# Attention and two feed-forward layers on one core: identity products in TensorE's prologue taken out

## What is computed

```python
q_d, k_d, v_d = means of q, k, v over groups of 4 positions
out_up    = repeat(softmax(scale * q_d @ k_d.T) @ v_d, 4)
scores    = where(|i - j| < 4, scale * q @ k.T, -1e9)
out_local = softmax(scores) @ v
x = (out_up + out_local) as (2304 tokens, 512)
h = relu(x @ w_in1)                 # 512 -> 2048
x = (h * h) @ w_out1                # 2048 -> 512
h = x @ w_in2
out = (relu(h) + log1p(exp(-|h|))) @ w_out2
```

## Time and profile before

| | |
|---|---|
| three runs | 908.38 to 908.83 us, median 908.71 |
| the profiled execution | 910.32 us, its span 908.5 us |
| TensorE matmul busy | 890.9 us, 98% of the span |
| VectorE, ScalarE, GpSimd busy | 612.3, 440.1 and 331.0 us |
| granted TensorE clock, mean | 0.988 of full |
| HBM read and written | 54.76 and 9.44 MB |

### The profile page before, as it was taken

One profiled execution on the slowest core, in us unless ns is written; L12 is line 12 of the kernel. 1 busy time (PEld: TensorE's weight loads), 2 busy tenths in 40 slices (PEclk: granted clock), 3 DMA queues, 4 the chain that ended last, 5 costly groups with the idle time before them and its releaser, 6 DMA issues.

```text
span 908.5 us, 14912 instructions
## 1 busy us (share of the span) xinstructions
PE 890.9 (98%) x5783; PEld 834.5 (92%) x5783; DVE 612.3 (67%) x1058; ACT 440.1 (48%) x1073; POOL 331.0 (36%) x160
## 2 busy tenths in 40 slices
PE   9979899999999999999999999999999999999998
PEld 7778799999999999999999999998999989999897
DVE  4579776876676766645245977777767767677675
ACT  5576355554646446453466634434434434434433
POOL 8699868788585975856100000000000000000000
PEclk9689999999999999999999999999999999999999
DMA  9670231231424221100155400200200200200000
GB/s 302 254 286 28 70 137 59 65 113 70 138 84 137 68 83 46 45 27 1 45 158 166 127 0 1 70 1 1 70 1 1 71 1 0 70 1 1 36 1 35
DMA packets 22037, 65.14 MB, mean 72 GB/s; under 512 B 2272, under 2 KB 9440, under 8 KB 21968
## 3 DMA queue, kind: packets, MB, share of 16 engines
q1 hardware_dynamic: 21968, 64.20, 21.0%
HBM read 54.76 MB, written 9.44 MB: 71 GB/s over the span
## 4 chain that ended last, share of the span: by engine, by line
PE 87%; POOL 6%; issue 2%; DVE 2%; ACT 1%; DMA 1%; SPq 0%; POOLq 0%; DVEq 0%
PE bank L1267 22%; PE bank L1281 22%; PE bank L680 20%; PE bank L649 20%; POOL w_lo L709 3%; POOL prod L451 2%; POOL prod L405 1%; PE bank L545 1%; DMA qk_first<-in_qk_grp 1%; PE bank L590 1%; PE bank L472 1%; PE bank L615 1%; PE bank L288 1%; DVE xs L482 0%; ACT bank L565 0%
## 5 line engine op out<-in xcount | busy, mean ns | idle before, releaser
L649 PE MATMUL bank<-x_hi,w_hi 128*128 128x288 f32 x512 | 157.6, 308 | 4.9 <-DVE g_lo L669 3.1
L451 POOL TENSOR_TENSOR prod<-sc,vt 128x1344 f32<-128x1344 f32 x42 | 134.9, 3235 | 60.0 <-DVE sc L439 52.4
L669 DVE TENSOR_TENSOR g_lo<-bank,g_hi 128x288 fp32r<-128x288 f32 x128 | 58.3, 456 | 144.5 <-ACT g_hi L664 144.4
L649 PE MATMUL bank<-x_lo,w_hi 128*128 128x288 f32 x512 | 152.2, 297 | 0.0
L649 PE MATMUL bank<-x_hi,w_lo 128*128 128x288 f32 x512 | 152.0, 297 | 0.0
L680 PE MATMUL bank<-g_hi,w_hi 128*128 128x288 f32 x512 | 150.9, 295 | 0.0
L680 PE MATMUL bank<-g_hi,w_lo 128*128 128x288 f32 x512 | 150.7, 294 | 0.0
L680 PE MATMUL bank<-g_lo,w_hi 128*128 128x288 f32 x512 | 150.6, 294 | 0.0
L995 ACT ACTIVATE sp_abs<-bank 128x384 f32<-128x384 f32 x96 | 46.9, 489 | 194.4 <-PE bank L1267 194.3
L405 POOL TENSOR_TENSOR prod<-qt,kt 128x1344 f32<-128x1344 f32 x42 | 130.7, 3118 | 17.9 <-DVE sc L412 12.3
L1267 PE MATMUL bank<-x_lo,w_hi 128*128 128x384 f32 x384 | 129.9, 338 | 0.0
(11 more groups left out here) (104 smaller groups left out, 1623.5 us busy)
## 6 DMA issues: line engine op xcount, KB each, us to landing
w_raw<-in_w SPq DMA_DIRECT2D x32, 512.0 KB, 4.2
qk<-in_qk_grp SPq DMA_DIRECT2D x12, 576.0 KB, 4.6
kt<-in_k_loc SPq DMA_DIRECT2D x7, 960.0 KB, 4.9
vt<-in_v_loc SPq DMA_DIRECT2D x7, 960.0 KB, 4.7
vg<-in_v_grp SPq DMA_DIRECT2D x16, 320.0 KB, 3.5
x_scratch<-ys SPq DMA_DIRECT2D x32, 144.0 KB, 3.1
x_raw<-x_scratch SPq DMA_DIRECT2D x6, 768.0 KB, 4.6
out<-y SPq DMA_DIRECT2D x18, 256.0 KB, 2.0
```

The lines of the kernel that those rows point to most:

```text
L451: nc.gpsimd.tensor_tensor(dst, pb, win, ALU.mult).then_inc(prod_ready[m % 2], 1)
L649: last = nc.tensor.matmul(h_ps[f % 2][:, 0:NT], w[:, f, wc], x[:, T % 2, kc], start=(kc == 0 and i == 0), stop=(kc == KC - 1 and i == 2))
L669: nc.vector.tensor_tensor(g_lo[:, f % 2], h_ps[f % 2][:, 0:NT], g_hi[:, f % 2].bitcast(F32), ALU.subtract).then_inc(g_ready, 1)
```

## The change

`keep_busy` and all its calls are taken out, and with them the argument `busy` of `first_x`. Every other instruction keeps its place in its engine's list. Since `first_x` had its fillers behind the waits for `x0_ready` and `up_ready`, those waits now stand directly before its own. In the changed file, code behind the function stands 5 or 6 lines higher.

```diff
@@ -282,11 +282,6 @@
             a.wait_ge(mask0_done, 2)
             nc.scalar.activation(mask0_r[0:BQ], mask0[0:BQ], ACT.Copy).then_inc(mask0_rounded, 1)
 
-        def keep_busy(pe, times):
-
-            for _ in range(times):
-                nc.tensor.matmul(X0[:, 0:P], ident[:], ident[:], start=True, stop=True)
-
         def first_scores(pe, j):
             pe.wait_ge(first_qk[j], 16)
             if j >= 2:
@@ -353,13 +348,12 @@
             for e in range(2):
                 nc.vector.tensor_copy(pT0[0:BK, j % 2, e], first_banks(j)[e][0:BK, 0:NT]).then_inc(pT0_copied, 1)
 
-        def first_x(pe, j, busy):
+        def first_x(pe, j):
 
 
             if j:
                 pe.wait_ge(x0_ready, j)
                 pe.wait_ge(up_ready, j)
-            keep_busy(pe, busy)
             if j == 0:
                 pe.wait_ge(v0_loaded, 16)
             pe.wait_ge(pT0_copied, 2 * j + 2)
@@ -1197,36 +1191,28 @@
         def _(pe):
             pe.wait_ge(ident_done, 2)
 
-            keep_busy(pe, 7)
             first_scores(pe, 0)
-            keep_busy(pe, 3)
             pair_scores(pe, 0)
-            keep_busy(pe, 6)
             first_scores(pe, 1)
-            keep_busy(pe, 4)
             first_turn(pe, 0)
-            keep_busy(pe, 1)
             pair_scores(pe, 1, (0,))
-            keep_busy(pe, 4)
             first_scores(pe, 2)
-            keep_busy(pe, 2)
             pair_turn(pe, 0)
-            keep_busy(pe, 3)
             pair_scores(pe, 1, (1,))
-            first_x(pe, 0, 5)
+            first_x(pe, 0)
             first_turn(pe, 1)
             pair_turn(pe, 1)
             pair_scores(pe, 2)
             first_scores(pe, 3)
             first_turn(pe, 2)
             pair_scores(pe, 3, (0,))
-            first_x(pe, 1, 0)
+            first_x(pe, 1)
             pair_turn(pe, 2)
             pair_scores(pe, 3, (1,))
             first_turn(pe, 3)
-            first_x(pe, 2, 4)
+            first_x(pe, 2)
             pair_turn(pe, 3)
-            first_x(pe, 3, 5)
+            first_x(pe, 3)
 
             hidden_in(pe, 0, 0)
             hidden_in(pe, 0, 1)
```

## The result

The changed kernel took 913.06 us in the median of 6 runs (912.01 to 914.64), the kernel before 908.41 us in 6 runs beside it (905.83 to 908.83). The ratio is 1.0053, interval 1.0034 to 1.0071: slower by 4.6 us, where 3.3 were forecast. The profiled execution took 912.71 us, its span is 910.9 us, 2.4 us longer than the span of before.

The account below looks back on a forecast made before the run. TensorE is packed from about 105 us, so prologue delay arrives whole. Steps after 10.2 us sum to 37.85 us, so `first_x(3)` ends at 48.0 instead of 44.7: 908.7 + 3.3 = 912.0 us, range 909.2 to 914.6.

Parts of the forecast that it names:

- The clock stays low without the early fillers: Prologue: with nothing dense before the hidden layer, TensorE's clock is low from 0; `first_turn(3)` comes 7 us late.
- Rival B: About even: clock rises once on scores of pair 2 and `first_scores(3)`; end at -1.5 to +0.8, 908.5 us; chance 0.12.
- The chain of steps: TensorE's prologue steps and copy waits after 10.2 us, at low clock: 37.85 us, `first_x(3)` ends at 48.0 instead of 44.7.
- The low start of the hidden layer (3 us) is paid before and after alike: Start of the hidden layer: 3 us at low clock in both kernels, so no difference from it.
- truly full about 3 us into the hidden layer: Sign in the changed kernel: TensorE's clock first reaches full about 3 us after the hidden layer begins.
- rival C: Slower: hidden layer stays low longer than 3 us, until 62 instead of about 51 us; +3 more, 915 us; chance 0.11.
- Late fillers "stand on the path" and only cost: Fillers in the low stretch: 2.0 us before `first_x(2)`, 2.4 us before `first_x(3)`, partly covering waits.
- Early fillers cost little at full clock: Prologue fillers at full clock fill time in which TensorE would wait for DMA, VectorE or ScalarE anyway.
- One for one downstream: After `first_x(3)`: its 3.3 us delay passes through VectorE's chain to 71.14 us and arrives at TensorE's end.
- the forecast 74.4: Sign in the changed kernel: GpSimd's first value product comes at 74.4 us, 71.14 before.
- The size: Whole kernel: +3.3 us, profiled execution from 910.32 to 913.6, median from 908.7 to 912.0 us.
- The rule on keeping TensorE busy: Skill rule: unbroken work reaches full clock; by it the prologue's real work raises it, -4 to -6, 904 us; chance 0.06.

Follow-up runs that it names:

- e3_first_seven: Only the first 7 of the 44 fillers left, at the head of TensorE's list, against the kernel before: 912.81 us, ratio 1.0036.
- e1_late_out: The 9 fillers at the heads of `first_x(2)` and `first_x(3)` out, 35 earlier ones kept, against the kernel before: 908.58 us, ratio 0.9993.
- e8_half: e5_hold with 24 early fillers in place of 35, measured against the kernel before: 904.21 us, ratio 0.9970.
- e5_again: e5_hold's kernel run once more to confirm it, against the kernel before: 905.03 us, ratio 0.9967.
- the second comparison: The changed kernel, all 44 fillers out, run once more beside the kernel before: 914.44 us, ratio 1.0049.
- e6_sixteen: Only the first 16 fillers (7, 3 and 6, up to `first_scores(1)`) left, against the kernel before: 912.01 us, ratio 1.0033.
- e5_hold: The 9 late fillers out, 35 early ones kept, 7 others put where TensorE stood idle, against the kernel before: 906.44 us, ratio 0.9967.

## Why the prediction was right, step by step

- **The clock stays low without the early fillers: right** in the trace and in 17 of 18 timed runs of the changed kernel, by their times (912 us or more). Rival B, given 0.12, is what the eighteenth did, and e3_first_seven's trace shows it too.
- **The chain of steps: right, 48.0 us forecast, 47.56 measured.** The single heads of the pair scores at low clock measure 1.07 to 1.17 us from start to start, where 1.13 was taken between 0.63 and 1.34. `first_scores` is 1.89, not 1.83: the row at 6.32 us had already caught the rise of the clock. One wait was counted too many: after `pair_turn(1)` the first head of `pair_scores(2)` needs no copy and goes at once (24.96 us). The copies of `pdT` cost 0.64, 0.59 and 0.99 us, not 0.92, 0.80 and 0.80. All four waits come to 2.2 us instead of 3.3. The other way went the load, at 10.43 instead of 10.21 us, and the scores of pair 2 with `first_scores(3)`, 3.37 us instead of 2.96. So a part of the agreement is luck: errors of up to 1.1 us cancelled to 0.4.
- **"The low start of the hidden layer (3 us) is paid before and after alike": wrong.** It lasted 5.0 us in the changed kernel against 2.8, about 1 us of TensorE's time more at half the clock, and the sign "truly full about 3 us into the hidden layer" failed. That is rival C's direction. It did no harm here, because TensorE stands idle 1.56 us before 58.81 us.
- **Late fillers "stand on the path" and only cost: wrong in general.** It was read from one execution, in which the clock had fallen before them. e1_late_out took them out: the path in its trace was shorter by 4.2 us, and the median gained nothing.
- **Early fillers cost little at full clock: nearly right.** Eleven fewer gave 0.6 us between the traces of e8_half and e5_again (1.0 us from `first_scores(1)` on), 0.8 us between their medians.
- **One for one downstream: right**, by the table. GpSimd's first value product came 0.9 us later than the forecast 74.4 without moving the end.
- **The size.** The sum came to +3.3 us, between the traces it is +2.8 us at the gate and +2.4 us in span. The medians differ by 4.6 us, because the trace of before was of its slower kind of execution: 910.32 us against a median of 908.4. The step "it becomes 913.6; the median is 1.6 lower; the forecast is 912.0" carried that 1.6 us over to the changed kernel. It had no such better kind of execution to bring its median down (912.71 in the profiled one, 913.06 in the median). Of the 4.6 us, that explains about two. In the second comparison the medians differ by 5.5 us, so the forecast's 912.0 us stood at the low side of what the change costs.
- **The rule on keeping TensorE busy** (the Trainium skill, "TensorE: Matmul & The Clock Gate", section "Why this matters for your kernels") told against the forecast. Stretches with no idle time stayed low here (19.31 to 34.15 us in the changed kernel), so being busy was not enough; two traces rose in such a stretch, so it is not excluded either.

## What to carry over

Work that nobody reads can be worth its time: here 44 dead products were worth about 5 us of 910, by the clock that they raised and held. Put it into idle time and not behind the wait of the work it precedes, and look at the end of the critical stage, not at busy shares, for what it does. Where a clock decides, one trace is one draw: look at the mean clock and the time of every run, together, before a term of the sum is read from a single profile, and compare the profiled execution's time with the median first.

## What the runs showed that was not expected

- The granted clock column reads 1.00 up to the first change on record, even where the matmuls run at 1.2 GHz: 1.34 us for the 12 records of L292 at 10.43 us with 1.00, against 0.77 at full clock.
- With transposes of the identity as fillers TensorE's clock rose and held as with products (e4_transposes, ratio 0.9996). The Trainium skill, same page, "Part 4: PE-mode transpose", says that transposes do not count as busy work in the same way; this run speaks against it, at least for float32 (the page's example is bf16).
- The clock fell after idle stretches that were each well under 1 us, among small products: 0.26, 0.86 and 0.34 us in e1_late_out, 0.78, 0.30 and 0.15 us in e6_sixteen. With seven fillers in such places it stayed full to the hidden layer in both traces, and 24 of 24 runs have a mean of 0.994 or more.
- The level at which a stretch begins matters: 30.79 to 44.68 us, with 0.13 us of idle time in it and 18 filler records, stayed low in the kernel before, while real work of the same kind from 19.48 to about 28 us, begun at full clock, kept it.
- The clock falls behind the prologue as well: in the trace of before it reads 0.68 from 60 to 64 us, in that of the changed kernel 0.79 from 64 to 72 us, in e5_hold's nowhere.
- The same kernel lies between 905.1 and 913.7 us over 93 runs, and its mean granted clock splits these runs into the two kinds told of above.
